# A third weight piece kept back: two 512 KB loads under way instead of three, from the fourth expert on

## The chip, the cores and the metric

The kernel runs on one core of one Trainium2 chip. The time is the device time of one execution in microseconds (us). The kernel before was run three times: 650.14, 652.07 and 654.15 us, median 652.07. The engines are named as in the profile: PE is TensorE's matmul, PEld its weight load, DVE is VectorE, ACT ScalarE, POOL GpSimd, SP SyncE; "SPq" or "ACTq" is the instruction queue of that engine, which also issues DMAs.

## The reference

Three layers follow each other over 2304 tokens of 512 features, all in float32:

```
x = attention(q, k, v)                      # 4 x 8 heads, 576 tokens, a window of 64
do = (x @ w_skip) > 0                       # tokens that go to an expert; the others pass
e_idx = argmax(x[do] @ w_gate)              # one of 8 experts each
for e in range(8):
    y[mask_e] = gate * (relu(x[mask_e] @ w1[e]) @ w2[e])     # 512 -> 1024 -> 512
x[do] = x[do] + y
h = x @ w_in                                # 512 -> 2048
out = (h * clip(h + 3, 0, 6) / 6) @ w_out   # 2048 -> 512
```

The weights of an expert are 2 MB (w1) and 2 MB (w2). The reference's inputs, computed on a host in the order in which the kernel takes the experts (the expert with index 4 first), send 291, 62, 83, 153, 108, 101, 35 and 59 tokens to them. In tiles of 64 tokens that is 5, 1, 2, 3, 2, 2, 1 and 1, in all 17 tiles.

## The kernel before

The kernel has three stages. The **attention** goes over 18 tiles of 128 tokens and routes each token: its row is scattered to a place in HBM (`x_rows`) that belongs to its expert. The **expert stage** goes over the 17 tiles of 64 rows, called g = 0 to 16 here. The **last layer** is 24 steps of matmuls (L1104, L1162).

In the expert stage PE does for each tile g, in this order: the first product with w1 (L1016, 128 matmuls), the transposition of the rows of tile g + 1 (L1008), and the second product with w2 (L1024, 32 matmuls). Three transfers go with each tile. ACT's queue issues the load of the rows of a tile ahead (`xin`, L543, two halves of 65 KB). POOL's queue issues an indirect scatter of the result `yo` of the tile before (L791). SP's queue issues the weights. The scatter of tile g - 1 is issued after PE's transposition for tile g + 1. DVE may write `yo` of tile g only when that scatter has landed (the wait ahead of L1806), and PE's second product of tile g + 1 waits for that write (L1812, through the wait in L1073) because both use one bank. PE's transposition waits for `xin` (L1069).

The weights of an expert lie in one of three slots of SBUF, expert e in slot e % 3. They come in eight **pieces** of 512 KB: four of w1 (128 rows of 4 KB each), four of w2 (rows of 2 KB). Piece n is 8e + c. `load_piece` (L328) issues a piece. Three semaphores `s_wp` take the pieces in turn, and before piece n is issued SP waits until piece n - 3 has landed, so that at most three are under way. Pieces 0 to 23 (experts 0 to 2) are issued during the attention and at the start of the expert stage. For each further expert e = 3 to 7, SP first waits until all tiles of expert e - 3 are done (L630), since it overwrites that expert's slot, and then issues its eight pieces. After the pieces of expert 7, SP waits for the last tile's row load (L638, L639) and issues the first loads of the last layer (L646, L591 to L599). PE waits for all pieces of an expert's w1 ahead of its first tile (L1057) and for those of its w2 ahead of the second product (L1072).

Of the kernel before, what the change touches and what calls it, by code (L numbers as in the profile page):

```python
# [5 lines left out]
def attention_moe_mlp_kernel(nc, q, k, v, moe_w_skip, moe_w_gate, moe_w1, moe_w2,  # L6
# [31 lines left out]
    DC = DM // P  # L38
    FC = F // P
    FC2 = F2 // P  # L40
    WQ = 3
# [20 lines left out]
    with ctx:  # L62
# [3 lines left out]
        def sem(name):  # L66
            return ctx.enter_context(nc.semaphore(name))
# [190 lines left out]
        s_wp = [sem(f"s_wp{i}") for i in range(WQ)]  # L258
# [68 lines left out]

        def load_piece(eng, n, dst, src):  # L328

            if n >= WQ:  # L330
                eng.wait_ge(s_wp[n % WQ], 16 * (n // WQ))
            eng.dma_start(dst, src).then_inc(s_wp[n % WQ], 16)

        def load_w1(eng, e):
# [9 lines left out]
        def piece_w1(eng, e, c):  # L344

            load_piece(eng, 8 * e + c, w1s[e % 3][:, c, :], moe_w1[SEQ[e], c * P:(c + 1) * P, :])

        def piece_w2(eng, e, c):

            rows = moe_w2[SEQ[e]].rearrange("(c p) f -> p c f", p=P)  # L350
            load_piece(eng, 8 * e + DC + c, w2s[e % 3][:, 2 * c:2 * c + 2, :], rows[:, 2 * c:2 * c + 2, :])
# [1639 lines left out]
```

## Time and profile before

| what | value |
|---|---|
| median of 3 runs | 652.07 us (650.14 to 654.15) |
| profiled execution, its own time | 651.28 us |
| span of the profiled execution | 649.5 us |
| PE busy | 627.4 us, 97% |
| granted PE clock, mean | 0.992 |
| DMA moved | 93.70 MB, mean 144 GB/s |
| share of DMA in the chain that ended last | 10% |

Times in the rows are us from the start of the span, unless marked ns. "[0.64 <-DVE yo L1812]" behind a row means that the engine was idle for 0.64 us ahead of it and that the named work ended that idle time, as inferred from semaphore events.

### The profile page before, as it was taken

The page shows a single profiled execution, that of the slowest core. Times are in us where ns is not written, and L with a number is a line of the kernel's source. Part 1 is how long each engine was busy: PE and PEld are TensorE (multiplying, and loading weights), DVE is VectorE, ACT ScalarE, POOL GpSimd, SP SyncE. Part 2 cuts the span into 40 slices and gives each one's busy share as a digit, 9 for nine tenths or more (in the row PEclk, how much of TensorE's full clock was granted, in tenths as well). Part 3 has the DMA queues.
Part 4 walks back from the last instruction along what each step waited for, and adds up shares of the span by engine and source line. Part 5 has one row for each costly group of instructions (what it writes and reads, how often), then busy time and mean ns, then how long its engine had stood idle before and what let it go on. Part 6 is the DMA issues. An engine that isn't in the chain of part 4 may idle for free.

```text
span 649.5 us, 17088 instructions
## 1 busy us (share of the span) xinstructions
PE 627.4 (97%) x6442; PEld 545.4 (84%) x6442; DVE 394.3 (61%) x1071; ACT 321.3 (49%) x674; POOL 87.8 (14%) x155
## 2 busy tenths in 40 slices
PE   7999996899999999999999999999999999999998
PEld 6788875778787788988888898888888988888886
DVE  3678886312111223787777688777776888777753
ACT  4899884111111233754444557544445574444433
POOL 5334443411111112000000004000000040000000
PEclk8999999899999999999999999999999999999999
DMA  9877998879986866312222226222222242222002
GB/s 168 166 181 173 232 279 286 276 249 308 328 316 222 290 240 191 97 51 81 82 83 65 66 66 204 73 82 81 83 66 65 66 150 78 66 68 70 26 0 98
DMA packets 115139, 93.70 MB, mean 144 GB/s; under 512 B 63676, under 2 KB 90816, under 8 KB 115072
## 3 DMA queue, kind: packets, MB, share of 16 engines
q1 hardware_dynamic: 105632, 79.80, 42.1%
q0 software_dynamic: 3408, 10.33, 4.2%
q10 hardware_dynamic: 6032, 2.68, 1.8%
q8 instruction: 42, 0.69, 0.4%
q14 instruction: 25, 0.20, 0.1%
HBM read 80.08 MB, written 13.11 MB: 143 GB/s over the span
## 4 chain that ended last, share of the span: by engine, by line
PE 81%; DMA 10%; SPq 2%; DVE 2%; issue 1%; another core or an unknown queue 1%; ACT 1%; ACTq 1%; POOLq 0%; DVEq 0%
PE bank L1162 31%; PE av L1104 28%; PE bank L1016 5%; PE av L1024 5%; DMA xin<-x_rows 4%; PE av L891 3%; DMA w2s<-in_moe_w 2%; DMA w1s<-in_moe_w 2%; PE bank L907 2%; SPq L517 2%; PE bank L847 2%; PE bank L832 2%; PE bank L937 1%; DMA x_rows<-yo,yrow 1%
## 5 line engine op out<-in xcount | busy, mean ns | idle before, releaser
L1162 PE MATMUL bank<-o_hi,g_lo 128*128 128x512 f32 x288 | 114.0, 396 | 0.0
L1162 PE MATMUL bank<-o_hi,g_hi 128*128 128x512 f32 x288 | 113.9, 395 | 0.0
L1162 PE MATMUL bank<-o_lo,g_hi 128*128 128x512 f32 x288 | 113.5, 394 | 0.0
L1104 PE MATMUL av<-xc_hi,w_hi 128*128 128x384 f32 x344 | 89.5, 341 | 0.0
L1104 PE MATMUL av<-xc_lo,w_hi 128*128 128x384 f32 x344 | 88.3, 337 | 0.0
L1104 PE MATMUL av<-xc_hi,w_lo 128*128 128x384 f32 x344 | 88.3, 337 | 0.0
L1878 DVE TENSOR_TENSOR g_lo<-act,g_hi 128x384 fp32r<-128x384 f32 x96 | 53.3, 556 | 43.6 <-ACT g_hi L1424 40.4
L1424 ACT CAST g_hi<-act 128x384 fp32r<-128x384 f32 x96 | 49.4, 515 | 51.4 <-DVE act L1871 49.3
L1104 PEld LDWEIGHTS av<-xc_hi,w_hi 128*128 128x128 f32 x344 | 63.0, 188 | 13.2 <-DVE act L1871 0.9
L1016 PEld LDWEIGHTS bank<-xeT,w1s 128*64 128x64 f32 x2176 | 69.0, 141 | 4.6 <-issue 2.4
L1414 ACT ACTIVATE rel<-hq,half 128x384 f32<-128x384 f32 x60 | 37.0, 617 | 70.4 <-DVE hq L1864 70.4
L1016 PE MATMUL bank<-xeT,w1s 128*64 128x64 f32 x2176 | 69.9, 225 | 1.2 <-issue 0.7
L1285 ACT ACTIVATE hT<-bank 128x128 f32<-128x128 f32 x68 | 18.9, 278 | 101.0 <-PE bank L1016 97.1
L1162 PEld LDWEIGHTS bank<-o_hi,g_lo 128*128 128x128 f32 x288 | 54.0, 188 | 13.0
L1024 PE MATMUL av<-w2s,hT 128*64 128x256 f32 x544 | 63.0, 382 | 1.2 <-DVE yo L1812 0.9
L1104 PEld LDWEIGHTS av<-xc_lo,w_hi 128*128 128x128 f32 x344 | 62.6, 188 | 0.2 <-DVE xc_lo L1842 0.2
L1104 PEld LDWEIGHTS av<-xc_hi,w_lo 128*128 128x128 f32 x344 | 62.4, 188 | 0.0
L1162 PEld LDWEIGHTS bank<-o_lo,g_hi 128*128 128x128 f32 x288 | 54.3, 188 | 6.5
L1806 DVE COPY yo<-xres 128x4 f32<-128x4 f32 x17 | 2.9, 169 | 93.2 <-DMA x_rows<-yo,yrow 93.2
L1162 PEld LDWEIGHTS bank<-o_hi,g_hi 128*128 128x128 f32 x288 | 54.0, 188 | 6.2
L1024 PEld LDWEIGHTS av<-w2s,hT 128*64 128x64 f32 x544 | 38.2, 137 | 21.2 <-issue 3.1
L1207 ACT ACTIVATE pr<-sm,mx 128x128 f32<-128x128 f32 x144 | 45.9, 395 | 3.8 <-DVE mx L1556 3.5
(188 smaller groups left out, 933.4 us busy)
## 6 DMA issues: line engine op xcount, KB each, us to landing
w1s<-in_moe_w SPq DMA_DIRECT2D x32, 512.0 KB
w2s<-in_moe_w SPq DMA_DIRECT2D x32, 512.0 KB
wor<-in_moe_w_out SPq DMA_DIRECT2D x24, 512.0 KB, 3.8
wir<-in_moe_w_in SPq DMA_DIRECT2D x24, 256.0 KB
wir<-in_moe_w_in SPq DMA_DIRECT2D x48, 128.0 KB
qraw<-in_q SPq DMA_DIRECT2D x36, 128.0 KB
vnow<-in_v SPq DMA_DIRECT2D x36, 128.0 KB
kraw<-in_k SPq DMA_DIRECT2D x34, 128.0 KB
```

Source lines behind the costliest of these rows:

```text
L517: eng.dma_start(dst[T % 3][W * x:W * x + W, :, :], tokens(src, 2 * T + x)).then_inc(s_load[T % 3], 16)
L832: last = pe.transpose(dst[:, pi * P:(pi + 1) * P], src[:, 2 * pi:2 * pi + 2, :].rearrange("p h d -> p (h d)"), ident[:, :])
L891: last = pe.matmul(av[x * W:(x + 1) * W, h // HP, at0:at0 + VW], prT[T % 2][:, h, x * W:(x + 1) * W], (vnow if x else vprev)[:, T % 3, h, ...
L1016: last = pe.matmul(into[x * W:(x + 1) * W, (f % 2) * ET:(f % 2 + 1) * ET], w1s[e % 3][:, c, cols:cols + W], xeT[:, c % 2, c // 2, :], star ...
L1024: last = pe.matmul(bank[6][x * ET:(x + 1) * ET, 0:DH], hT[:, f, :], w2s[e % 3][:, f, x * DH:(x + 1) * DH], start=(f == 0), stop=(f == FC - 1))
L1104: last = pe.matmul(into[:, 0:GN], a[it % 2][:, W_AT[w], c, :], b[:, X_AT[x], c, :], start=(n == 0 and fresh), stop=(n == 3 * XQ * len(pair ...
L1162: last = pe.matmul(bank[tile][:, :], a[c][:, i * P:(i + 1) * P], b[it % 2][:, units(it)[c], :], start=(p == 0 and c in (0, 2) and n == 0), ...
L1207: last = sc.activation(pr[T % 2][:, h, :], sm[:, h, :], ACT.Exp, scale=-1.0, bias=mx[T % 2][:, h:h + 1])
L1285: sc.activation(hT[:, 2 * m:2 * m + 2, :], into[:, 0:2 * ET].rearrange("p (f s) -> p f s", f=2), ACT.Relu).then_inc(s_hc, 1)
L1414: sc.activation(rel[n % 2][:, :], quarter(it, c), ACT.Relu, scale=1.0 / 6.0, bias=half[:, :]).then_inc(s_rel, 1)
L1424: sc.copy(g_hi[c][:, :], act[n % 2][:, :]).then_inc(s_ghi, 1)
L1878: dve.tensor_tensor(g_lo[c][:, :], act[n % 2][:, :], g_hi[c][:, :].bitcast(fp32), ALU.subtract).then_inc(s_glo, 1)
```

## The change

Pieces 0 to 23 (`3 * (DC + FC // 2)` is 24) go as before. From piece 24, the first of the fourth expert, `ahead` is 2: piece n waits for piece n - 2. The semaphore on which a piece counts, and the waits of PE for the weights, stay.

```diff
         def load_piece(eng, n, dst, src):
 
-            if n >= WQ:
-                eng.wait_ge(s_wp[n % WQ], 16 * (n // WQ))
+            ahead = WQ if n < 3 * (DC + FC // 2) else WQ - 1
+            if n >= ahead:
+                eng.wait_ge(s_wp[(n - ahead) % WQ], 16 * ((n - ahead) // WQ + 1))
             eng.dma_start(dst, src).then_inc(s_wp[n % WQ], 16)
```

## Rows read from the trace of the kernel before

**Rows 1.** The page, engines: busy time, share of the span, instructions.

```profile
PE 627.4 (97%) x6442; PEld 545.4 (84%) x6442; DVE 394.3 (61%) x1071; ACT 321.3 (49%) x674; POOL 87.8 (14%) x155
```

**Rows 2.** Windows: stretch, PE, PEld, DVE, ACT, POOL busy (instructions), clock, DMA share, GB/s.

```profile
158.90:204.40 45.50, 43.57 (x942) 36.26 (x940) 7.76 (x32) 8.87 (x30) 4.87 (x5) 1.00 0.88 305
...
207.80:223.40 15.60, 15.13 (x322) 12.37 (x320) 2.36 (x8) 4.00 (x12) 1.95 (x2) 1.00 0.86 293
223.80:239.50 15.70, 15.62 (x337) 12.77 (x334) 3.67 (x12) 4.95 (x13) 1.95 (x2) 1.00 0.86 301
239.50:243.50 4.00, 4.00 (x126) 3.76 (x123) 2.32 (x6) 1.18 (x5) 0.00 (x0) 1.00 0.03 6
```

**Rows 3.** Timeline of PE: start, duration, instruction, count, idle time before.

```profile
154.79 0.44 PE L1008 MATMUL av<-ident,xin 128*128 128x128 f32 x2 [0.18 <-DMA xin<-x_rows]
...
162.49 0.44 PE L1008 MATMUL av<-ident,xin 128*128 128x128 f32 x2
...
171.32 3.67 PE L1024 MATMUL av<-w2s,hT 128*64 128x256 f32 x32 [0.64 <-DVE yo L1812]
...
182.53 3.90 PE L1016 MATMUL bank<-xeT,w1s 128*64 128x64 f32 x128
...
187.45 3.81 PE L1024 MATMUL av<-w2s,hT 128*64 128x256 f32 x31 [0.24 <-DMA w2s<-in_moe_w]
...
220.07 3.67 PE L1024 MATMUL av<-w2s,hT 128*64 128x256 f32 x32 [0.28 <-DVE yo L1812]
...
246.83 4.11 PE L1016 MATMUL bank<-xeT,w1s 128*64 128x64 f32 x128
250.88 0.44 PE L1008 MATMUL av<-ident,xin 128*128 128x128 f32 x2
251.24 3.67 PE L1024 MATMUL av<-w2s,hT 128*64 128x256 f32 x32
```

**Rows 4.** Timeline of SP's queue, merged: start, length, issues in it.

```profile
158.96 3.83 SPq L332 DMA_DIRECT2D w1s<-in_moe_w  x4
163.83 6.56 SPq L332 DMA_DIRECT2D w2s<-in_moe_w  x4
...
193.73 4.43 SPq L332 DMA_DIRECT2D w2s<-in_moe_w  x4
207.83 3.89 SPq L332 DMA_DIRECT2D w1s<-in_moe_w  x4
...
223.85 3.92 SPq L332 DMA_DIRECT2D w1s<-in_moe_w  x4
228.86 6.55 SPq L332 DMA_DIRECT2D w2s<-in_moe_w  x4
243.52 1.44 SPq L646 DMA_DIRECT2D xn<-x_rows  x3
```

**Rows 5.** Line 332 from 155 to 240: duration of an issue, ns min/median/max.

```profile
L332 SPq DMA_DIRECT2D w2s<-in_moe_w x20: 367/373/379, 163.8 to 235.0; - x20
```

**Rows 6.** The chain that ended last: start, duration, what.

```profile
158.96 3.48 DMA w1s<-in_moe_w
162.46 5.36 DMA w1s<-in_moe_w
...
197.33 6.22 DMA xin<-x_rows
```

**Rows 7.** Timeline of POOL: the scatters of yo.

```profile
163.91 0.97 POOL L791 DMA_INDIRECT x_rows<-yo,yrow  x1 [6.75 <-PE av L1008]
...
204.99 0.97 POOL L791 DMA_INDIRECT x_rows<-yo,yrow  x1 [7.47 <-PE av L1008]
```

**Rows 8.** Timeline of DVE: the copies that wait for the scatter, the writes of yo.

```profile
170.40 0.17 DVE L1806 COPY yo<-xres 128x4 f32<-128x4 f32 x1 [7.10 <-DMA x_rows<-yo,yrow]
...
186.74 0.47 DVE L1812 SCALAR_TENSOR_TENSOR yo<-av,xres 128x256 f32<-128x256 f32 x1
...
207.47 0.17 DVE L1806 COPY yo<-xres 128x4 f32<-128x4 f32 x1 [2.67 <-DMA x_rows<-yo,yrow]
```

## The prediction, made before the changed kernel was run

> **What bounds the kernel now.** I read the page first: PE is busy for 627.4 of 649.5 us [rows 1]. A change of loads can only win what PE idles, or lose by making PE idle. The change acts from piece 24, which SP issues at 158.96 [rows 4]; the last piece is issued in the row that begins at 228.86. So the stretch that can move is 158.9 to about 255, until the last second product begins at 251.24 [rows 3].
>
> The windows show PE's idle time there. It is 45.50 - 43.57 = 1.93 us while the pieces of experts 3 to 5 flow, 0.47 us for expert 6, 0.08 us for expert 7 and nothing in the gap after [rows 2]. That is 2.48 us. DMA is busy for 0.88, 0.86 and 0.86 of the three bursts and for 0.03 of the gap, so the idle time comes with the bursts. The granted clock is 1.00, the upper level, in all of them, and stays out of the sum.
>
> Then the timeline of PE, for what ends those waits. One tile takes 162.49 - 154.79 = 7.70 us when nothing is late; the twelve periods from 154.79 to 250.88 take 96.09 us, which is 3.69 us over 12 x 7.70 [rows 3]. The wait of 0.64 us ahead of 171.32 is for DVE's write of `yo`; the chain shows `xin` taking 6.22 us from its issue at 197.33 [rows 6]. One row misleads: at 187.45 it names a weight piece. Tile g = 8 (the second product at 187.45) is the first of expert 3 by the counts 5, 1, 2, all of whose pieces were issued before 170.4 [rows 4]. DVE's write of `yo` ended at 186.74 + 0.47 = 187.21 [rows 8], 0.24 us before PE began, and I take that as the releaser. **No PE wait in this stretch is for weights; they are for the small transfers beside them.**
>
> **The change, part by part.** It adds no instruction. It replaces 40 waits by 40 stricter ones. It has two effects.
>
> *First, the weights come more slowly.* The first piece of the burst lands 3.48 us after its issue (the fourth issue waits for it, at 162.46) [rows 6]; the second lands at 163.83, when the fifth is issued [rows 4], 1.37 us later. With three under way, the last piece of expert 5 is issued at 193.73 + 4.43 - 0.37 = 197.79 [rows 4, 5]. It waited for the 21st of the burst, so 20 pieces took 197.79 - 162.46 = 35.33 us, 1.77 us each. The trace has no long stretch with two under way, so I bound it. A lone piece spends 3.48 - 1.37 = 2.11 us outside the transfer itself. With two under way a piece then takes max(1.77, (2.11 + 1.77) / 2) = 1.94 us. The lower end is 1.77 (the queue was full enough anyway). The upper end is a latency that stays as it is with three, 3 x 1.77 = 5.31, which gives 5.31 / 2 = 2.65 us. I take 2.0, near the worked-out value, since a lone piece (3.48) is nearest to what each piece would see with one ahead of it.
>
> At 2.0 us: expert 3's last piece lands at 162.46 + 7 x 2.0 = 176.5, and w1 is needed at 182.53, w2 at 187.45 [rows 3]. Cover: 6 us and more. Expert 5's last piece lands at 162.46 + 23 x 2.0 = 208.5. Expert 6 may start at 207.83, when tile 10 is done, as before; expert 7 at 223.85, when tile 12 is done [rows 4]. In that last burst the first piece lands at 227.44 (223.85 + 3.92 less an issue of about 0.33), the last at 227.44 + 7 x 2.0 = 241.4. Its w1 is needed at 246.83 and its w2 at 251.24. Queued behind the pieces on SP are the first loads of the last layer, which begin at 243.52 [rows 4]; the last piece would be issued at 227.44 + 5 x 2.0 = 237.4 instead of 235.0. POOL's and ACT's queues have no new wait. So this effect costs nothing on the path, covered by 6 us on SP and 10 us on PE.
>
> *Second, one piece less stands beside the small transfers.* The scatter issued at 163.91 let DVE go at 170.40, after 6.49 us, with three pieces under way; the one issued at 204.99, with none, after 2.48 us [rows 7, 8]. The scatter goes out 163.91 - 162.49 = 1.42 us after the transposition starts; the next transposition can start 7.70 us later; the second product 0.36 us after that (250.88 to 251.24); from DVE's copy to that product 171.32 - 170.40 = 0.92 us pass. So a scatter up to 7.70 + 0.36 - 0.92 - 1.42 = 5.7 us old costs nothing. If one piece less takes 1.77 us off 6.49, 4.7 remain and the wait is gone. For `xin` 6.22 would become 4.5, also under what the period allows (issued at 197.33 for a transposition that can start about 202.9, 5.5 us). The bounds of the gain: nothing, where the small transfers do not feel the depth of SP's queue; at most the 3.69 us over the pure period. Of the 2.48 us idle I count 1.8, between the share that the waits for `yo` make (0.64, 0.24 and 0.28 [rows 3], 1.16) and all of it: the bursts get longer, 7 x 0.23 = 1.6 us for each short one and 23 x 0.23 = 5.3 us for the long one, so one tile more runs beside a burst, at 2.48 us over some ten such tiles, 0.25 us each.
>
> **The sum.** The profiled execution took 651.28 us, 0.8 under the median of 652.07: 651.28 + 0 - 1.8 = 649.5, and against the median 652.07 - 1.8 = 650.3.
>
> **The rivals.**
> (a) *The small transfers don't get faster.* They stand in the queues of ACT and POOL, not behind SP's pieces; it would be enough for one piece to be there at all times to slow them as much. Against it: 2.48 us with no piece. For it: with three pieces under way a latency near 5 us occurs too: the chance of hitting a busy moment may count for more than the depth. Then nothing is gained, and the longer bursts put one or two tiles more beside them: 0.3 to 0.5 us more. Time: 652.4. The Trainium skill (DMA: Bandwidth & Descriptors, Queues, rings and completion order) has each DMA engine go round between the queues for which it has work; by that rule the number waiting in SP's queue would not matter to the others, and this rival would be the outcome.
> (b) *The weights become the bound: slower.* The place is the last burst. If the latency of a piece does not fall with only two under way, the pieces come every 2.65 us and the bursts run into each other without a gap: the last issue at 162.46 + 37 x 2.65 = 260.5, 17 us after 243.52; the last piece lands at 162.46 + 39 x 2.65 = 265.8, 14.6 us after 251.24. Price about 15 us, time 667. It decides from (243.52 - 162.46) / 37 = 2.19 us a piece for SP's next loads, from (251.24 - 162.46) / 39 = 2.28 us for w2; each 0.1 us beyond costs about 4 us. For it: landings do need all parts of a piece, and 5.36 us is seen for one [rows 6]. Against it: that latency includes two pieces ahead, which by 1.37 us each leave 2.6 to 4.
> (c) *It does nothing:* if the third piece never helped nor hurt, both effects are zero, time 652.1. The row at 158.96 shows three issued together and the fourth held for 3.48 us, so the limit does act; this falls together with (a) in time.
>
> **How the numbers follow.** The forecast (a gain of 0.8 to 3 us) gets 0.55, (a) and (c) together 0.33, (b) 0.12, a third of it (0.04) beyond 1%, since 1% needs more than 2.28 + 6.5 / 39 = 2.45 us a piece. The three runs differ by 4 us, so a median may stand 1 to 1.5 us off by itself. The range goes from 648.4 (the full 3.69 us), less 1 for the runs, 647.4, to 652.4 plus 1.5 for the runs and a first part of (b), 655. A difference under 1%, 6.5 us, can't be told from no change here: within 1% 0.93, slower 0.05, faster 0.02, since the whole idle time to be won is 0.6% of the time.
>
> **What would show it.** SP's issues from piece 26 on come one by one, the third of each burst only some 3.5 us after the first; the spacing is about 2.0 us (1.9 to 2.15), the long burst is issued until about 204.5 instead of 197.8, the last piece at about 237. The scatters and `xin` in the bursts take at most 5.7 us, and PE's idle time from 158.9 to 243.5 falls from 2.5 to about 0.7 us; the stretch after 255 keeps its length. The forecast is wrong if the spacing is over 2.2 us, if a PE wait ahead of L1016 or L1024 is truly for an expert's first piece, or if scatters still take 6.5 us with two pieces under way.

## The result, and the profile after

The changed kernel takes 656.68 us (median of 11 runs, 655.19 to 661.28), the kernel before 652.07 us (median of 11 runs). The ratio is 1.0059, 95% interval 1.0033 to 1.0085: **3.9 us slower (2.2 to 5.5)**, where 1.8 us faster was forecast. The two medians by themselves are 4.6 us apart; where they differ I go by the ratio, which has an interval. The profiled execution has a span of 654.9 us, 5.4 us more than before.

First the windows of the changed kernel, in the stretches of [rows 2] and the one after them. The columns are those of [rows 2].

```profile
158.90:204.40 45.50, 45.50 (x970) 37.46 (x966) 8.06 (x33) 8.88 (x30) 5.46 (x6) 1.00 0.78 254
...
207.80:223.40 15.60, 14.19 (x280) 11.29 (x278) 2.56 (x10) 3.72 (x11) 1.95 (x2) 1.00 0.78 254
223.80:239.50 15.70, 15.70 (x342) 12.93 (x338) 3.67 (x12) 4.94 (x13) 1.95 (x2) 1.00 0.79 252
239.50:243.50 4.00, 4.00 (x118) 3.62 (x114) 1.66 (x4) 1.48 (x5) 0.00 (x0) 1.00 0.81 271
243.50:254.80 11.30, 7.46 (x160) 6.01 (x156) 3.08 (x10) 1.48 (x5) 1.94 (x2) 1.00 0.74 231
```

Two things stand here at once. In the long stretch PE has no idle time left (45.50 of 45.50, before 43.57). And the gap of DMA after 239.5 is gone: its share is 0.81 there, before 0.03. The weights now flow without a break, at 254 GB/s instead of 305.

SP's queue (timeline, merged) shows the same from the issuing side; the three rows behind it are SP's waits from 155 to 262, by line and by what it waited for (us in total, times, longest):

```profile
160.34 5.25 SPq L333 DMA_DIRECT2D w1s<-in_moe_w  x4
167.86 7.70 SPq L333 DMA_DIRECT2D w2s<-in_moe_w  x4
...
204.86 7.98 SPq L333 DMA_DIRECT2D w2s<-in_moe_w  x4
214.90 7.54 SPq L333 DMA_DIRECT2D w1s<-in_moe_w  x4
...
234.34 7.34 SPq L333 DMA_DIRECT2D w1s<-in_moe_w  x4
243.00 8.63 SPq L333 DMA_DIRECT2D w2s<-in_moe_w  x4
253.04 1.29 SPq L647 DMA_DIRECT2D xn<-x_rows  x3
```

```profile
SPq L333 <- DMA w1s<-in_moe_w: 38.6, 18, 3.4
SPq L333 <- DMA w2s<-in_moe_w: 32.0, 18, 3.2
SPq L320 <- PE av L1025: 5.6, 1, 5.6
```

Expert 6 begins at 214.90 and expert 7 at 234.34 (before 207.83 and 223.85 [rows 4], when their slots became free). SP reaches the first loads of the last layer at 253.04, before at 243.52. SP waits for PE once (L320), ahead of 160.34; from there on each piece waits only for the landing of an earlier one. **So from 160.34 on PE can't hold up the stream of weights.**

The timeline of PE, with the rows that answer to [rows 3] and the new idle times:

```profile
156.07 0.44 PE L1009 MATMUL av<-ident,xin 128*128 128x128 f32 x2 [0.22 <-DMA xin<-x_rows]
...
171.95 3.67 PE L1025 MATMUL av<-w2s,hT 128*64 128x256 f32 x32
...
202.40 0.44 PE L1009 MATMUL av<-ident,xin 128*128 128x128 f32 x2
...
206.27 3.31 PE L1017 MATMUL bank<-xeT,w1s 128*64 128x64 f32 x106
211.00 0.86 PE L1017 MATMUL bank<-xeT,w1s 128*64 128x64 f32 x22 [1.41 <-issue]
211.79 0.44 PE L1009 MATMUL av<-ident,xin 128*128 128x128 f32 x2
...
250.48 0.92 PE L1017 MATMUL bank<-xeT,w1s 128*64 128x64 f32 x24 [0.80 <-issue]
251.33 0.44 PE L1009 MATMUL av<-ident,xin 128*128 128x128 f32 x2
255.07 5.36 PE L1025 MATMUL av<-w2s,hT 128*64 128x256 f32 x32 [3.30 <-DMA w2s<-in_moe_w]
260.36 1.53 PE L1092 MATMUL bank<-ident,xn 128*128 128x128 f32 x12
```

Six tiles in a row, from 156.07 to 202.40, take 46.33 us, 7.72 each: no wait for rows or scatters. At 255.07 PE begins the last second product 3.30 us late. Here the row's releaser is right: the tile is the only one of expert 7, and the chain of waits shows its last piece issued at 251.26 (once the piece of 245.80 had landed) and landing as PE starts (its first row is the second piece of the long burst):

```profile
160.73 4.52 DMA w1s<-in_moe_w
...
245.80 5.44 DMA w2s<-in_moe_w
...
251.26 3.69 DMA w2s<-in_moe_w
...
255.07 5.36 PE av L1025 x32
```

That product then takes 5.36 us instead of 3.67. The windows of the wait and of the product give the reason in the clock, the third number from the end:

```profile
251.80:255.10 3.30, 0.03 (x2) 0.04 (x2) 0.00 (x0) 0.37 (x1) 0.97 (x1) 1.00 0.66 189
255.10:260.40 5.30, 5.30 (x33) 3.10 (x33) 0.29 (x2) 0.00 (x0) 0.00 (x0) 0.68 0.99 316
```

PE stood still for 3.3 us, and in the 5.3 us after it the granted clock averaged 0.68, so part of them ran at the lower level (1.2 GHz instead of 2.4). From 260.40 to 265.00 it is 1.00 again.

**The balance of this pair of profiles** goes from the transposition in tile 4 (154.79 before, 156.07 after) to the first transposition of the last layer (254.85 and 260.36): 100.06 and 104.29 us, +4.23.

| part | before | after | difference |
|---|---|---|---|
| ten of the twelve tile periods, over 7.70 us each | 3.37 | 0.14 | -3.23 |
| the two periods that end in tile 11 and in tile 16, over 7.70 us; in the changed kernel they hold the gaps marked as issue | 0.32 | 2.72 | +2.40 |
| from the last of these transpositions to the last layer | 3.97 | 9.03 | +5.06 |

The first two lines are the twelve periods, 96.09 and 95.26 us. The third is 3.30 of waiting, 1.69 of slow clock and 0.07 beside.

The table says where the time lies, not what set it. The last product starts when the last piece has landed, and PE can't hold up the pieces. So in the changed kernel nothing that PE wins or loses ahead of that product moves its start: the 3.23 us won and the 2.40 us of gaps only made the wait longer or shorter. Counted from the transposition in tile 4, the last product starts 99.00 us later (255.07 - 156.07), in the kernel before 96.45 us later (251.24 - 154.79). **The +4.23 are 2.55 us, by which the stream of weights is longer than the work that PE had to do before, and 1.69 us of slow clock.**

The rest of the difference of the two spans, about 1.2 us, arose before 156.07, where the kernels are the same.

### The profile page after: what moved, and what is told of

Read it like the earlier page. It is cut to its first block, busy times and chain, and to the rows that moved or that the text cites. A ratio compares the mean times of both kernels' runs of the same rounds, so it can differ in the third digit from the quotient of the medians.

```text
span 654.9 us, 17088 instructions
## 1 busy us (share of the span) xinstructions
PE 630.0 (96%) x6442; PEld 547.2 (84%) x6442; DVE 393.8 (60%) x1071; ACT 321.1 (49%) x674; POOL 87.7 (13%) x155
## 4 chain that ended last, share of the span: by engine, by line
PE 76%; DMA 18%; ACT 2%; issue 1%; DVE 1%; another core or an unknown queue 1%; ACTq 1%; SPq 0%; POOLq 0%; DVEq 0%
PE bank L1163 31%; PE av L1105 28%; DMA w1s<-in_moe_w 7%; DMA w2s<-in_moe_w 7%; PE bank L848 3%; PE av L892 3%; PE bank L908 3%; DMA xin<-x_rows 2%; PE bank L833 2%; PE av L1025 2%; PE bank L1017 2%; PE bank L938 1%; DMA x_rows<-yo,yrow 1%; PE bank L923 1%; PE av L1092 1%
## 5 line engine op out<-in xcount | busy, mean ns | idle before, releaser
L1025 PE MATMUL av<-w2s,hT 128*64 128x256 f32 x544 | 64.4, 390 | 3.5 <-DMA w2s<-in_moe_w 3.3
```

The lines of the kernel that those rows point to most:

```text
L1025: last = pe.matmul(bank[6][x * ET:(x + 1) * ET, 0:DH], hT[:, f, :], w2s[e % 3][:, f, x * DH:(x + 1) * DH], start=(f == 0), stop=(f == FC - 1))
```

## Experiments

Ratios are those of the time to the kernel before in runs on the same chip, with 95% intervals; the two second profiles are single runs and have none. Since the time before tile 4 scatters (its transposition starts between 153.4 and 158.5 in the twelve profiles), I also give two lengths from each profile: the *twelve periods* (transposition in tile 4 to that in tile 16, 92.4 us if nothing is late) and the *stretch* (transposition in tile 4 to the last layer; 96.4 us if nothing is late).

| kernel | twelve periods | stretch | ratio |
|---|---|---|---|
| before | 96.09 | 100.06 | 1 |
| before, second profile | 94.19 | 98.17 | |
| changed | 95.26 | 104.29 | 1.0059 (1.0033 to 1.0085) |
| changed, second profile | 94.59 | 100.71 | |
| two under way for experts 3 to 5 only | 98.27 | 102.24 | 1.0014 (0.9993 to 1.0035) |
| two under way for experts 6 and 7 only | 95.48 | 99.45 | 1.0014 (0.9985 to 1.0043) |
| four under way | 97.13 | 101.11 | 1.0010 (0.9989 to 1.0030) |
| four halves under way | 94.10 | 98.07 | 0.9996 (0.9970 to 1.0021) |
| no weights of experts 3 to 7 | 92.44 | 96.42 | 0.9951 (0.9928 to 0.9974) |
| two under way, half the bytes | 92.97 | 96.95 | 0.9952 (0.9933 to 0.9972) |
| five halves under way | 95.22 | 99.19 | 0.9980 (0.9966 to 0.9993) |
| four halves, from the third expert | 93.87 | 97.84 | 0.9987 (0.9968 to 1.0007) |

**Which of the two effects is real?** The two kernels that decide it were these.

*No weights of experts 3 to 7.* It leaves out their 40 pieces and PE's waits for them, and computes with what lies in the slots.

```diff
         def wait_pieces(eng, n):
 
+            n = min(n, 24)
...
         def load_piece(eng, n, dst, src):
 
+            if n >= 24:
+                return
             if n >= WQ:
                 eng.wait_ge(s_wp[n % WQ], 16 * (n // WQ))
```

> Leaves out the weights of experts 3 to 7: their 40 pieces are not loaded and PE does not wait for them, so those products use what lies in the slots. It bounds what weights under way cost the small transfers. Theory A: from the transposition in tile 4 to that in tile 16 twelve periods of 7.70 us, 92.4 us instead of 96.1 before, no wait for row loads or scatters; the time falls by 3 to 4 us, ratio 0.994 to 0.996. Rival (the waits of before come from something else, such as HBM latency of the scatters): the periods stay near 8 us and the ratio at 1.000.

The ratio is 0.9951 (0.9928 to 0.9974), 3.2 us faster, and the windows of its profile have no idle PE at all:

```profile
158.90:204.40 45.50, 45.50 (x968) 37.44 (x966) 8.18 (x33) 8.88 (x30) 5.23 (x6) 1.00 0.13 36
204.40:243.50 39.10, 39.10 (x818) 32.04 (x816) 8.58 (x28) 10.41 (x30) 5.32 (x6) 1.00 0.12 33
243.50:254.80 11.30, 11.30 (x197) 8.96 (x194) 3.24 (x11) 2.26 (x7) 1.49 (x2) 1.00 0.80 260
```

So 3.2 us (1.7 to 4.7) is all that the weights of these experts cost before. It bounds what any version of this change can win.

*Two under way, half the bytes.* The waits of the changed kernel, but each piece from 24 on loads only its first 256 KB. The edit is against the changed kernel.

```diff
+            if n >= 24:
+                dst, src = (t[:, 0:F // 2] if len(t.shape) == 2 else t[:, 0:1, :] for t in (dst, src))
+            ahead = WQ if n < 24 else WQ - 1
```

> Two pieces under way from the fourth expert as in the changed kernel, but each piece loads only its first half (256 KB); the other half of each slot keeps old data. It takes away the lateness and keeps two under way. Theory A: the stream needs about 1.7 to 1.9 us a piece, every burst ends long before its weights are needed, no wait for w2 and no slow clock at the end, periods of 7.70 us: ratio 0.994 to 0.997. If two under way cost something apart from lateness, the time stays above before, ratio 1.002 or more.

The ratio is 0.9952 (0.9933 to 0.9972). Two under way without lateness win the whole bound; the changed kernel with the same waits and twice the bytes is at 1.0059. The distance, 0.0107 or 7.0 us, is what the late weights cost: the loss of 3.9 us and the 3.2 us that PE wins and then spends waiting. This run alone can't say whether the waits for rows and scatters went because of the number under way or of the bytes, since 0.5 MB is under way here, not 1 MB; the first tiles of the changed kernel, which have 1 MB, show no such wait either.

**Is the result the same in a second profile?**

> The changed kernel once more, for a second profile. Theory A: pieces again every 2.3 to 2.4 us in one stream from 160 to 255, PE waits 2.5 to 4 us for the last w2, its second product of the last tile then runs at the lower clock (5.4 instead of 3.7 us). The two gaps inside first products (1.4 and 0.8 us, which no wait explains) may move or vanish if they are chance; if they belong to the change they come back in the first tile of expert 4 and of expert 7.

The changed kernel took 655.56 us this time. Its pieces were issued from 161.61 to 250.43 (242.40 + 8.40 - 0.37), 2.28 us each over 39 steps, in the first profile 2.33. PE waited for w2 again, for 2.08 us, and both gaps came back, in the same tiles:

```profile
207.54 3.31 PE L1017 MATMUL bank<-xeT,w1s 128*64 128x64 f32 x106
211.99 0.86 PE L1017 MATMUL bank<-xeT,w1s 128*64 128x64 f32 x22 [1.14 <-issue]
...
251.18 0.92 PE L1017 MATMUL bank<-xeT,w1s 128*64 128x64 f32 x24 [0.43 <-issue]
252.03 0.44 PE L1009 MATMUL av<-ident,xin 128*128 128x128 f32 x2
254.54 3.67 PE L1025 MATMUL av<-w2s,hT 128*64 128x256 f32 x32 [2.08 <-DMA w2s<-in_moe_w]
258.15 1.53 PE L1092 MATMUL bank<-ident,xn 128*128 128x128 f32 x12
```

The slow clock did not come back: the product took 3.67 us. The expectation of 5.4 us was wrong: the lower clock came after 3.3 us of standing still in the first profile and did not come after 2.1 us in this one.

> The kernel before once more, for a second profile: pieces every 1.75 to 1.9 us, PE idle 2 to 3 us from the fifth tile to the last for row loads and scatters, none of 0.7 us or more inside a first product if such gaps belong to the longer stream.

The kernel before took 653.17 us. Its twelve periods exceed 92.4 by 1.79 us here, 3.69 in the first profile, and there is one gap marked as issue of 0.32 us. So what can be won differs from run to run by 2 us; the 3.2 us above come from many runs.

**Where do two under way cost, and where not?** Two kernels took the change apart by stretch: `ahead` is `WQ - 1 if 24 <= n < 48 else WQ` in the first and `WQ - 1 if n >= 48 else WQ` in the second.

> Two pieces under way for experts 3 to 5 only (pieces 24 to 47), three again for experts 6 and 7. Theory A (two effects: waits for the small transfers vanish, and at 2.36 us a piece the stream runs late only at its end): the stream of experts 3 to 5 ends near 217, expert 6 follows without a gap at about 1.8 us a piece and ends near 231, expert 7 near 246, so PE never waits for w2 in the last tile. PE's idle time beside experts 3 to 5 falls from 1.9 us to under 0.5 us. Time 1.5 to 2.5 us below before (ratio 0.996 to 0.998). Rival B (two under way is dearer wherever it is used): time 2 us or more above before, since 24 of the 40 pieces are still slowed.

Neither theory's ratio was met. It is 1.0014 (0.9993 to 1.0035): theory A's 0.996 to 0.998 is excluded, and B's 1.003 and more lies at the edge of the interval. In the profile the first part came as theory A has it: the six periods from 154.04 take 46.6 us together, 0.4 over 6 x 7.70, and the pieces of experts 3 to 5 are issued at 158.21 to 210.89, 2.29 us apart. Expert 6 started at 211.95 instead of 207.83 and the stream then ran on at three under way without a gap. The last six periods have 51.7 us, 5.5 us too many: waits for rows and scatters (0.35, 0.22, 0.28, 0.26, 0.56) and again the two gaps, here 0.87 and 1.41 (the second is in these rows):

```profile
246.69 3.36 PE L1017 MATMUL bank<-xeT,w1s 128*64 128x64 f32 x101
251.46 0.92 PE L1017 MATMUL bank<-xeT,w1s 128*64 128x64 f32 x24 [1.41 <-issue]
252.31 0.44 PE L1009 MATMUL av<-ident,xin 128*128 128x128 f32 x2
252.68 3.67 PE L1025 MATMUL av<-w2s,hT 128*64 128x256 f32 x32
```

PE did not wait for the last w2 (3.67 us, no idle time before it), which was theory A's point. What was won in the first half was lost in the second; here PE's last product waits for nothing, so the gaps do cost their length.

> Three under way for experts 3 to 5 as before, two for experts 6 and 7 only. Theory A: expert 6 starts at 207.8 and ends near 228, expert 7 ends near 246, both bursts have a gap of their own, w2 of expert 7 is in time (needed near 250). Only the 0.5 us of waits beside these bursts goes: ratio 0.998 to 1.001. Rival B: the slow end belongs to these bursts themselves, PE waits for the last w2 as in the changed kernel: ratio 1.003 to 1.006.

The ratio, 1.0014 (0.9985 to 1.0043), does not decide between 0.998 to 1.001 and 1.003 to 1.006. The profile does: the transposition at 252.60 is followed by the product at 252.97, so w2 was in time, and the four periods before the last have 7.70 or 7.71 us. Rival B, which wanted the wait for w2 here, falls. One gap of 0.70 us stands in the last tile.

**Does a deeper queue slow the small transfers?** From the fourth expert on, four semaphores `s_lp` of their own and four pieces under way:

```diff
+        LQ = 4
...
+            for half in range(1):
+                h = 1 * (n - 24) + half
+                if h >= LQ:
+                    eng.wait_ge(s_lp[h % LQ], 16 * (h // LQ))
...
+                eng.dma_start(half_of(dst, half), half_of(src, half)).then_inc(s_lp[h % LQ], 16)
```

(`half_of` returns the whole piece here.)

> From the fourth expert on four pieces of 512 KB under way instead of three, on four semaphores of their own. Theory A (small transfers are slowed by what stands in SP's queue): scatters and row loads in the bursts take longer than the 6.5 us of before, PE idles 4 us or more in 158.9 to 243.5 instead of 2.5: ratio 1.002 to 1.005. Rival C (the DMA engines go round between queues, the depth of SP's queue does not matter as long as it isn't empty): latencies of 4 to 6.6 us as before, ratio 1.000.

The ratio, 1.0010 (0.9989 to 1.0030), decides nothing. In the profile PE's idle time is 3.36 us (2.37 before, by the same count) and the longest single waits for row loads are 0.83 and 0.91 us (0.67 before), less than the 4 us that theory A gave. Against a spread of 2 us between two profiles of one kernel that is weak support for A. The scatters say more. From POOL's issue to DVE's copy, those issued while SP was issuing pieces took 6.2 us in the mean here (six, 5.6 to 6.8), in the kernel before 5.8 and in its second profile 5.2 (seven each). That is theory A's direction and not rival C's. The pieces came every 1.48 us (from 161.29 to 195.44, 23 steps), before every 1.69 us by the same count, so three under way did not reach the highest rate either.

**Bytes or pieces?** The late pieces go as two halves of 256 KB, on four (or five) semaphores:

```diff
+            for half in range(2):
+                h = 2 * (n - 24) + half
+                if h >= LQ:
+                    eng.wait_ge(s_lp[h % LQ], 16 * (h // LQ))
...
+                eng.dma_start(half_of(dst, half), half_of(src, half)).then_inc(s_lp[h % LQ], 16)
```

> From the fourth expert on each piece goes as two halves of 256 KB, four halves under way: the same 1 MB under way as in the changed kernel, in four parts. Theory A with the bytes as the cause of the small transfers' delay: PE waits for row loads and scatters are gone as in the changed kernel (idle under 0.7 us), and since a landing frees 256 KB instead of 512 KB the DMA engines idle less: 1.9 to 2.1 us for each 512 KB instead of 2.36, so the last w2 is in time. Time 2 to 3 us below before (ratio 0.995 to 0.997). If the rate with 1 MB under way is given by the bytes alone (1 MB in 4.7 us), the halves still come at 2.36 us per 512 KB and the time is that of the changed kernel, ratio 1.006.

With the same 1 MB under way as in the changed kernel, all halves were issued from 161.93 to 245.27 (236.72 + 8.92 - 0.37), 2.11 us per 512 KB against 2.33, and in the stretch PE waited for no weights, rows or scatters:

```profile
242.55 0.44 PE L1030 MATMUL av<-ident,xin 128*128 128x128 f32 x2
...
246.65 3.07 PE L1038 MATMUL bank<-xeT,w1s 128*64 128x64 f32 x93
250.60 1.25 PE L1038 MATMUL bank<-xeT,w1s 128*64 128x64 f32 x33 [0.88 <-issue]
251.79 0.44 PE L1030 MATMUL av<-ident,xin 128*128 128x128 f32 x2
252.16 3.67 PE L1046 MATMUL av<-w2s,hT 128*64 128x256 f32 x32
```

Eleven of twelve periods lie between 7.70 and 7.78 us. The rate and the absence of waits are as theory A had them, and 0.9996 instead of 1.0059, with as many bytes under way, shows that it was the rate that made the changed kernel slow. The scatters beside the halves took 4.9 us in the mean, beside the two whole pieces of the changed kernel 4.7: the same bytes, the same delay. The size was missed: 0.9996 (0.9970 to 1.0021) is not the 0.995 to 0.997 expected. The last period has 9.24 us, so the gap in the last tile takes 1.5 us of it; why the rest is missing I can't say.

> As the kernel with four halves of 256 KB under way from the fourth expert on, but five (1.25 MB). If bytes under way set both the rate and the delay of the small transfers, this lies between four halves (2.13 us per 512 KB, no wait beside the bursts) and three whole pieces (1.8 us, 1 to 2.5 us of waits): 1.9 to 2.0 us per 512 KB, waits of 0 to 1 us, ratio to before 0.997 to 1.000. If the number of transfers counts and not their bytes, the waits are back to 2 to 4 us and the ratio is 1.000 to 1.003.

Five halves: 1.85 us per 512 KB (158.54 to 202.08, 47 steps), waits of 0.20 and 0.29 us beside the first burst, and 0.9980 (0.9966 to 0.9993), within what the bytes theory gave. **This version beats both kernels**, by 1.3 us (0.5 to 2.2) the one before. Only the timed runs show it: the stretch of its one profile, 99.19 us, lies between the two of the kernel before. The gap in its last tile is 1.65 us.

> Four halves of 256 KB under way already from the third expert on (piece 16). The burst of that expert ends about 1 us later (from 154 on all of it is landed, it is needed at 167), and the row load and scatter of tiles 2 to 4 stand beside 1 MB instead of 1.5 MB. The wait for row loads ahead of tile 5 (0.2 to 1.5 us in the profiles so far, with 0 to 1.9 us where no weights follow) comes mostly from the first loads of the last layer, which go unlimited behind that burst, so it stays: ratio to before 0.996 to 0.999, within 0.2% of the kernel that begins with the fourth expert.

The ratio is 0.9987 (0.9968 to 1.0007), as expected. It can't be told from the kernel that begins with the fourth expert (0.9970 to 1.0021), nor from the kernel before.

## Why the prediction was wrong

**The step that failed is the spacing of the pieces: "I take 2.0, near the worked-out value, since a lone piece (3.48) is nearest to what each piece would see with one ahead of it."** The trace after has 2.36 us: the second piece, issued at 160.73, landed 4.52 us later at 165.25, the last at about 255.0, 38 pieces later. With two under way that is a latency of 4.7 us each. A lone piece was the wrong neighbour. The row that shows a piece with one ahead of it is the second of each burst: issued right behind the first, it lands at 163.83 [rows 4], some 4.5 us after its issue (the burst begins at 158.96, an issue takes 0.37). Half of 4.5 is 2.25, beyond the 2.19 that rival (b) named for SP's next loads and just under its 2.28 for w2. The term that was mis-sized is the latency in the model behind 1.94: 2.11 us outside the transfer and 1.77 us for it, 3.88 in all, where 4.7 was measured. DMA's share fell from 0.88 to 0.78 in the same stretch, so time is lost between the pieces; the four halves, which ask for the next 256 KB as soon as 256 KB have landed, got part of it back. Nor was the spacing even: 2.27 us for experts 3 to 5 and 2.42 for the last 16 pieces (212.47 to 251.26), in the second profile 2.22 and 2.35. Why the later ones are slower is open; the last product stood at their end.

- **Weights slower (effect one): direction right, size wrong.** The sum "at 2.0 us" left gaps between the bursts; at 2.36 there are none. The prediction's own formula then gives 162.46 + 39 x 2.36 = 254.5 for the last piece, 3.3 us after 251.24; PE waited 3.30 us. That the two agree so well is partly luck, since PE's own time ahead of that product also moved, by -3.23 and +2.40 us. Rival (b)'s mechanism is what happened, at 2.36 instead of 2.65 us a piece, and it got a chance of 0.12.
- **SP's next loads: the threshold of 2.19 us counted for nothing.** They began 9.5 us later (253.04) and PE did not wait for them in this profile; in the second it waited 0.18 us. The 11.3 us that lay between their issue and their first use before (243.52 to 254.85) were cover that the prediction did not count; 7.3 us of it were left (253.04 to 260.36), 5 of these through the late last product itself.
- **Small transfers (effect two): the waits went as forecast, but each transfer gained less, and the kernel could not use it.** The waits fell by 3.23 us in this pair; the kernel without these weights wins 3.2 us in the timed runs, and the one with half the bytes wins all of that. In the changed kernel the gain went into the wait for w2. The size per transfer, 1.77 us, was too large. In the changed kernel the scatters issued at 180.69 and 196.09 let DVE go at 185.77 and 201.11, after 5.1 and 5.0 us, that of 165.29 after 5.4 and that of 236.29 after 5.55 (the first fence is POOL's timeline, the second DVE's):

```profile
165.29 0.97 POOL L792 DMA_INDIRECT x_rows<-yo,yrow  x1 [6.86 <-PE av L1009]
...
180.69 0.97 POOL L792 DMA_INDIRECT x_rows<-yo,yrow  x1 [6.73 <-PE av L1009]
...
236.29 0.97 POOL L792 DMA_INDIRECT x_rows<-yo,yrow  x1 [6.73 <-PE av L1009]
```

```profile
170.68 0.17 DVE L1807 COPY yo<-xres 128x4 f32<-128x4 f32 x1 [6.13 <-DMA x_rows<-yo,yrow]
...
185.77 0.17 DVE L1807 COPY yo<-xres 128x4 f32<-128x4 f32 x1 [6.71 <-DMA x_rows<-yo,yrow]
...
241.84 0.17 DVE L1807 COPY yo<-xres 128x4 f32<-128x4 f32 x1 [7.02 <-DMA x_rows<-yo,yrow]
```

  The prediction took its 6.49 us from one of the longest. Scatters issued while SP was issuing pieces took in the mean, from POOL's issue to DVE's copy:

| under way in SP's queue | mean, us | longest, us |
|---|---|---|
| nothing (no weights of experts 3 to 7; tiles 5 to 14) | 2.8 | 3.3 |
| 0.5 MB in two parts | 3.8 | 4.4 |
| 1 MB in two parts (changed; second profile) | 4.7; 4.8 | 5.6; 5.6 |
| 1 MB in four parts | 4.9 | 5.9 |
| 1.25 MB in five parts | 5.2 | 6.4 |
| 1.5 MB in three parts (before; second profile) | 5.8; 5.2 | 6.6; 5.9 |
| 2 MB in four parts | 6.2 | 6.8 |

  So one piece less took 0.4 to 1.1 us off the mean. The two kernels that change over within a run agree: 5.0 us with two under way and 5.9 with three in the one, 5.8 with three and 5.0 with two in the other. It was enough, since the longest fell under the 5.7 us that the period allows; only what is over that line costs anything.
- **Rival (a) falls:** neither its 652.4 us nor its mechanism came. By the Trainium skill's rule (DMA: Bandwidth & Descriptors, Queues, rings and completion order: an engine goes round between the queues that have work) as the prediction read it, the number waiting in SP's queue would not matter to the scatters. In these traces their delay follows the bytes under way there.
- **Missing from every case: the gaps inside first products.** They make 2.4 us in the table of the first pair, though there the wait for w2 would have taken their place; where no such wait follows (two under way for experts 3 to 5, four or five halves) they cost their length. Expert 4's gap (1.41, 1.14, and 0.87 with two under way for experts 3 to 5) appears in three profiles, and in none of the nine others. The one in the last tile is in eight of the twelve, from 0.27 to 1.65 us. DMA's queues show single packets of the instruction queue (16 KB), here in 206 to 210 us after, and in 196 to 198 before:

```profile
q8 instruction: 1, 0.02, 1.6%
```

```profile
q8 instruction: 1, 0.02, 4.8%
```

  In all twelve profiles such a packet can be placed near these two products (in windows of 0.1 us). In the eleven products with a gap it begins 1.0 to 2.5 us after the product (208.4 against 206.27, and 248.2 against 246.47 in the changed kernel); in the thirteen without one it begins at most 1.0 us after it, or earlier (197.4 against 207.56, and 247.8 against 246.83 before). At the border the two can hardly be told apart: no gap at 0.97 us, one of 0.27 us at 1.03. That PE waited for its own instructions, which came late, fits all of these places. (The small gap of 0.32 us in a second product, in the second profile of the kernel before, has a packet 2.3 us ahead of it too, at 190.5.) It is only argued: no run set out to move the packet, and why it comes early or late isn't known. The cause stays open.
- **The slow clock** (1.69 us) was in no case either. It followed the wait and came in one of two profiles.

In sum, the stream of weights, at 2.36 instead of 2.0 us a piece, ended 2.55 us after the point where PE's last product had begun before (both counted from tile 4), and the slow clock added 1.7: +4.2 in the pair of profiles. In the second pair of profiles the stretch grew by 2.5 us; the timed runs say +3.9.

## What to carry to other kernels

A cap on transfers under way trades the worst latency of everything beside them for their own rate; before lowering it, take the rate from a row where exactly that many were under way, and compare it with the rate at which the last buffer is needed, not with the slack of the first. Once an engine waits for that buffer, whatever it saves before the wait is lost in it. Where the rate has no slack, lower the bytes per transfer instead of their number: five halves of 256 KB under way kept most of the rate (1.85 against 1.69 us per 512 KB), removed most of the waits, and gave the one version that is measurably faster, 0.9980. A latency beside the critical path costs only what exceeds its period: look at its longest values, not at its mean.

## What the runs showed of the hardware that was not expected

- A 512 KB load took 3.5 us with none ahead of it and 4.7 us in a stream with one other under way. The time per 512 KB was 1.48, 1.69, 1.85, 2.09 and 2.27 us with 2, 1.5, 1.25 (halves), 1 (halves) and 1 MB under way, from the first to the last issue for experts 3 to 5 (second profiles: 1.80 with 1.5 MB, 2.22 with 1 MB); the two last differ only in how finely the same 1 MB is cut.
- An indirect scatter from another queue took 2.8 us with none of these loads under way, 3.8 with 0.5 MB, 4.7 to 4.9 with 1 MB, in two parts or four, 5.2 to 5.8 with 1.5 MB and 6.2 with 2 MB.
- After 3.3 us without a matmul the granted clock averaged 0.68 over the next 5.3 us, and 32 matmuls took 5.36 instead of 3.67 us; after 2.1 us in another profile it stayed at 1.00.
- PE stood still for up to 1.65 us inside a product without a wait, after 93 to 106 of the 128 matmuls of the first product of expert 4 or of expert 7, always when a packet of the instruction queue had begun 1.0 to 2.5 us into that product.
